# Second mixing: x2 loads behind u's landed store, and the last batch's turned rows on ScalarE's queue

## The reference

```
kv  = k^T v per head;  out = q kv;  x = out / rms(out) * g_norm           # linear attention
th  = x w_theta;  u = x + w_tok_r (x cos th) + w_tok_i (x sin th)         # first mixing
x2  = u + relu(u w_ch)
h   = relu(x2^T w_tok1) w_tok2;  u2 = x2 + h^T                            # second mixing
out = u2 + relu(u2 w_ch1) w_ch2                                           # channel products
```

## Time and profile before

| what | value |
|---|---|
| median of three runs | 1176.14 us |
| profiled execution, its own time | 1176.91 us |
| its span | 1175.1 us |
| TensorE busy | 1154.3 us, 98% |
| VectorE, ScalarE, GpSimd busy | 71%, 41%, 28% |
| granted TensorE clock | full in the whole span |

### The profile page before, as it was taken

How to read it: one execution, slowest core, us unless ns; L and a number is a source line. 1 busy time by engine, 2 the same in 40 slices (tenths; PEclk the granted TensorE clock), 3 DMA queues, 4 the chain that set the end, 5 groups by cost and what they waited for, 6 DMA issues and landing times.

```text
span 1175.1 us, 20563 instructions
## 1 busy us (share of the span) xinstructions
PE 1154.3 (98%) x7790; PEld 1116.7 (95%) x7790; DVE 834.9 (71%) x1243; ACT 481.0 (41%) x758; POOL 327.9 (28%) x210
## 2 busy tenths in 40 slices
PE   5999999999999999999999999999999999999998
PEld 5799999999999999999988999999999999999998
DVE  3968878686969687777557667667666786666664
ACT  3623425141424233334343555555556543333331
POOL 4462434444353534331552313214200000000000
PEclk9999999999999999999999999999999999999999
DMA  9714526160625330319997888666768999999983
GB/s 278 197 28 107 122 69 133 44 144 13 164 38 149 52 80 0 83 42 303 332 310 279 280 310 272 266 238 242 286 229 312 397 300 293 262 252 307 296 207 54
DMA packets 327383, 228.25 MB, mean 194 GB/s; under 512 B 231440, under 2 KB 295312, under 8 KB 326288
## 3 DMA queue, kind: packets, MB, share of 16 engines
q1 hardware_dynamic: 324912, 227.03, 63.3%
q10 hardware_dynamic: 2400, 0.30, 0.2%
HBM read 136.84 MB, written 92.80 MB: 195 GB/s over the span
## 4 chain that ended last, share of the span: by engine, by line
PE 86%; DMA 5%; DVE 3%; SPq 2%; issue 1%; POOL 1%; ACT 1%; DVEq 0%; ACTq 0%; POOLq 0%
PE bank L43 10%; PE bank L45 10%; PE bank L44 10%; PE bank L1377 10%; PE bank L1379 10%; PE bank L1378 10%; PE bank L367 6%; PE bank L373 6%; PE bank L368 6%; DMA u_scratch<-attention_u 3%; PE bank L312 3%; PE bank L326 1%; PE bank L282 1%; DMA attention_g<-g_scratch 1%; DVE attention_u L1268 1%
## 5 line engine op out<-in xcount | busy, mean ns | idle before, releaser
L367 PE MATMUL bank<-weights_tok,z_z 128*128 128x288 f32 x576 | 164.3, 300 | 0.3
L368 PE MATMUL bank<-weights_tok,z_z 128*128 128x288 f32 x576 | 161.2, 294 | 0.0
L373 PE MATMUL bank<-weights_tok,z_z 128*128 128x288 f32 x576 | 125.0, 295 | 0.8 <-POOL z_z L965 0.6
L367 PEld LDWEIGHTS bank<-weights_tok,z_z 128*128 128x128 f32 x576 | 108.1, 188 | 1.2 <-issue 1.1
L368 PEld LDWEIGHTS bank<-weights_tok,z_z 128*128 128x128 f32 x576 | 108.1, 188 | 0.0
L948 POOL TENSOR_TENSOR weights_rms_inverse<-weights_mean_squares,weights_minus_half 128x8 f32<-128x8 f32 x40 | 66.4, 1662 | 114.2 <-DVE weights_mean_squares L725 114.0
L373 PEld LDWEIGHTS bank<-weights_tok,z_z 128*128 128x128 f32 x576 | 92.5, 187 | 1.3 <-POOL z_z L965 0.8
L596 ACT ACTIVATE weights_x_channel_major<-attention_u 128x288 fp32r<-128x288 f32 x64 | 28.5, 446 | 139.0 <-DVE attention_u L792 139.0
L43 PE MATMUL bank<-weights_x_channel_major,weights_ch 128*128 128x288 f32 x256 | 77.4, 302 | 0.0
L963 POOL TENSOR_TENSOR z_z<-tokens_cos,z_z 128x512 fp32r<-128x512 f32 x24 | 31.9, 1329 | 159.8 <-ACT z_z L589 143.8
L45 PE MATMUL bank<-weights_x_channel_major,weights_ch 128*128 128x288 f32 x256 | 75.4, 294 | 0.0
(11 more groups left out here) (297 smaller groups left out, 3589.7 us busy)
## 6 DMA issues: line engine op xcount, KB each, us to landing
g_scratch<-attention_staged SPq DMA_DIRECT2D x36, 960.0 KB, 3.9
weights_g<-g_scratch SPq DMA_DIRECT2D x24, 1152.0 KB, 10.6
g_scratch<-attention_staged SPq DMA_DIRECT2D x36, 384.0 KB, 4.7
x_scratch<-attention_u SPq DMA_DIRECT2D x8, 1152.0 KB, 4.5
u_scratch<-attention_u SPq DMA_DIRECT2D x16, 576.0 KB, 7.6
weights_raw_u<-u_scratch SPq DMA_DIRECT2D x6, 1536.0 KB, 7.7
qkv_u_left<-u_scratch SPq DMA_DIRECT2D x12, 768.0 KB, 10.1
x_tokens_scratch<-z_x_turned SPq DMA_DIRECT2D x112, 72.0 KB, 2.0
```

The source lines that it names most:

```text
L367: pe.matmul(out, x, wtok[0][:, zt, hs], start=(i == 0), stop=False)
L368: pe.matmul(out, x, wtok[1][:, zt, hs], start=False, stop=False)
L373: mm = pe.matmul(tok_bank(b, g)[:, 0:HALF], z[1][:, zt, c * P:(c + 1) * P], wtok[0][:, zt, half * HALF:(half + 1) * HALF], start=False, st ...
```

## The change

SyncE waits, before it loads x2 of batch n + 2, until the second half of u2 of batch n has landed. The turned rows of the last batch are no longer stored from SyncE behind x2 but from ScalarE, in the same batches 1, 2 and 3, behind the conversions of the `w_ch1` parts. The first four transfers stay on SyncE.

```diff
@@ phase_b, sync
             if n + 2 < B:
+                sp.wait_ge(s_st[1], DMA * (n + 1))
                 load(sp, n % 2, n + 2)
-            if 1 <= n < NC:
-                store_last_turned(sp, n)
@@ phase_b, scalar, batch(n)
             for step in range(len(UP_ORDER)):
                 if UP_BATCH[step] == n:
                     up_hi(step)
+            if 1 <= n < NC:
+                store_last_turned(act, n)
             if n == B - 2:
                 act.wait_ge(g_w, len(UP_ORDER))
```

## The result

The changed kernel takes 1183.42 us in the median (four runs, 1181.89 to 1184.46), the kernel before beside it 1176.21. The ratio is 1.0061, with a 95% interval of 1.0044 to 1.0079: slower by 7.2 us, above the range of 1174.6 to 1181.2. The profiled execution took 1183.27 us, its span is 1181.5.

A forecast was written before the change was run, and what follows sets the result against it. TensorE, with 2.2 us of waits on the single-u-buffer store loop, was taken to bound the kernel. Batch terms of + 0.3, + 0.2, + 1.15, - 0.45 and + 0.4 gave 1176.14 + 1.6 = 1177.7 us; range 1174.6 to 1181.2.

The forecast's parts named there:

- What bounds the kernel: Second mixing: TensorE's weight loads wait 2.2 us for the residual, all the change can give back; the single-u-buffer loop delays it.
- At most 13.2: TensorE's own need in us between residual 0 of batches 5 and 6; the loop is slower by about half a microsecond.
- The issues on ScalarE: Twelve turned-row stores, four each in batches 1 to 3, at 0.56 us an issue; TensorE's 0.9 us stall costed at nothing.
- the cover: Batch 2's residual 0 waits for the store until 576.86 anyway, hiding ScalarE's delay; if held, some 5.6 us late.
- rival 3: ScalarE held by its four issues over 4 us in batch 1, hidden values late: 1179 to 1183, chance 0.13.
- rival 2: Loop slower than taken: turned rows 1 us a turn, x2 1.5 us: 1179 to 1182, chance 0.25.
- The late x2 loads: x2 loads, held for the store's second half, delay tokens and stores 0.4 to 1.5 us a turn; 0.7 taken.
- A store without x2 behind it: What an emptier queue may give the store of u: taken as nothing, with 1 us a turn as other end.
- Rival 1: Store lands within 7 us of issue without x2 beside it, in batches 1 to 4: 1173.9 to 1175, chance 0.2.
- The turned rows off SyncE: Token loads behind the turned rows on SyncE issue faster, 0.77 + 0.73 = 1.5 us gone in two turns.
- The turned rows beside the store: ScalarE's turned-row transfers, beside u's stores in batch 1, cost the loop 0 to 1.7 us per four; 0.3 taken.

The follow-up runs named there:

- second experiment: The changed kernel with the added wait taken out, so the x2 loads don't wait and ScalarE still stores the turned rows: 1179.83 us, ratio 1.0026.
- third experiment: The changed kernel with ScalarE's turned stores one batch later, in batches 2, 3 and 4, wait kept: 1179.05 us, ratio 1.0025.
- fifth experiment: The changed kernel with ScalarE's turned stores in batches 2, 3 and 4 and no wait ahead of the x2 loads: 1175.15 us, ratio 0.9991.
- store-first kernel: The kernel before, with the first half of u stored ahead of the token load in each batch: 1180.06 us, ratio 1.0038.
- fourth experiment: The changed kernel, but the x2 load issued in batch 4 doesn't wait: 1180.28 us, ratio 1.0036.
- first: The changed kernel with the turned rows back on SyncE, behind the waiting x2 loads: 1187.1 us, ratio 1.0089.

## Why the prediction was wrong

**What bounds the kernel** was right: TensorE's waits of 2.2 us were all there was to gain, and the loop over the single u buffer is what any delay goes through. The best version found gains 1.9. "At most 13.2" a batch for TensorE was a bound; it needs 12.75, so the loop was slower than TensorE by 0.7 us a turn on average, not by half a microsecond.

**The issues on ScalarE were costed at nothing; this is the step that failed.** It had two parts. The price was taken from where the engines had room (0.56 us each, ending at 572.4), although the moment in question has the token load's 1.3 MB in flight. The row for the full queue, 8.16 us for four, was at hand and nearer to that state; the true hold is 6.2 us. The text argued that ScalarE's own queue starts empty. It does, and three stores went in within 2.6 us; the fourth didn't. The DMA view shows why the empty queue didn't help: between 568.9 and 573.0 us not one packet of ScalarE's queue moved, and from 573.0 to 573.5 a single one; the engines were on SyncE's queue. The second part was the cover, residual 0 of batch 2 at 576.86 by the store; with the hold it came at 579.82, released by TensorE. It was bounded at 5.6 us late and is 2.9. This is rival 3, its mechanism and place as described, given 0.13. The forecast had it begin at 570.17, behind the conversion; the issues began at 568.96, with it. The rivals were priced one at a time. The second experiment comes closest to rival 3 alone, 1179.83, and the third to rival 2 alone, 1179.05; both came, and the changed kernel is above the range of either.

**The late x2 loads: mechanism right, term mis-sized.** 0.7 us a turn was taken. In the changed kernel the landings in batches 3 and 4 are 8.0 and 7.9, just 7.3 + 0.7; in batch 5 it is 9.98. With the third experiment's 7.9, 9.0, 9.4 and 8.6 the term is 0.6 to 2.1 us, mean 1.4 against 7.3; not all of it is the wait's, since in batches 3 and 4 the fifth experiment's kernel, which is the third's without the wait, took 8.1 and 7.6 where the third's took 9.0 and 9.4. Its upper end was in the text: batch 4's second half landed 2.5 us behind the first before too, and that row was set aside for the milder one. In a loop that has used up its lead the worst turn counts.

**A store without x2 behind it: rightly nothing.** Rival 1 is refuted by the changed kernel itself: with no x2 behind the stores of batches 2 to 5 they landed in 7.6 to 10.0 us, none sooner than in the same batch before (7.1 to 7.6). The store-first kernel says why. The Trainium skill's rule of a receipt that takes up to 2 us at high load (DMA: Bandwidth & Descriptors, Latency and other measured facts) would, by the forecast's estimate, have given the store up to 1.8 us back; with the tokens behind it in the queue it took 3.5 us against 3.0 alone, so here load behind it accounts for 0.5; no run measures the receipt by itself.

**The turned rows off SyncE** saved the issuing they were said to: 0.38 us for every first token load, 1.5 us in two turns. What the text had not seen is that they are worth far more once the wait is there: 10.8 against 7.2 us.

**The turned rows beside the store** were given 0.3 us a turn. By the Trainium skill's rule that an engine goes round between its queues packet by packet (DMA: Bandwidth & Descriptors, Queues, rings and completion order) they would, as the forecast read it, have overtaken the stores. In batch 1 they did not; the changed kernel's landing times of the four there and of the store beside them:

```profile
u_scratch<-attention_u SPq DMA_DIRECT2D x1, 576.0 KB, 9.1
...
x_tokens_scratch<-ttention_x_turned_last ACTq DMA_DIRECT2D x4, 72.0 KB, 9.2
```

Their median is 9.2 us, as long as the store. The store beside them took about 1 us more than before (8.07). In the kernels of the third and fifth experiments, with no turned rows in that batch, it took 8.2 and 8.5, so the rows' own share is between 0.6 and 1 us, more than the 0.3 taken; the store was not what residual 0 waited for in that batch, so this changed nothing.

**The clock was not in the sum.** A stop of TensorE was costed at its length. In the changed kernel's profiled execution one was followed by 3.4 us at the lower level, worth 1.7 us, about as much as the whole forecast.

## What to carry to other kernels

In these kernels a transfer lands by what is queued ahead of it; a wait that holds back a transfer behind it gives it next to nothing and pushes the held one in front of the next urgent one. Reorder or cut the transfers ahead instead, and check that the consumer of the moved one has the time. Before DMA issues are moved to a computing engine, look at how many its queue takes while the DMA engines are full and what that engine owes next; three were free here and the fourth cost 3.5 us. Where a loop has little lead, size a delay by its worst turn, and count a stop of TensorE with the clock that follows it.

## What the runs showed of the hardware

- ScalarE's DMA issues don't wait for the activation in front of them: in the changed kernel the first was issued at 568.96, in the same moment as the 1.49 us conversion that precedes it in program order, and in batch 2 before that conversion (576.83, the conversion at 579.06).
- With the DMA engines full, a fourth store of 72 KB in pieces of 128 bytes held its issuing engine for 3.63 us, behind 0.45, 0.61 and 1.41 for the first three; in the second and fourth experiments' kernels it was 4.39 and 4.05. In each of them the first packet of ScalarE's queue moved about 3.5 to 4.5 us after the first issue. Whether the count, the bytes or the pieces set the limit, no run separates. On SyncE, in the kernel before, one of such four took up to 3.8 us as well.
- After stops of TensorE of 2.0 to 3.7 us the granted clock fell to 1.2 GHz for 3.4 us in four kernels (changed, first, second and fourth experiment); after other stops of 2.0 us (third experiment) and 3.6 us (changed kernel, batch 1) it did not. What decides is open.
- A store's landing follows what is ahead of it in its queue: 576 KB took 3.0 us alone, 3.2 to 3.6 in five of six batches with tokens, a store and x2 behind it, 4.4 to 6.1 with 512 KB of tokens ahead, and 7.1 to 8.1 with all the tokens ahead.
